# Routing inside the delta rule, fixed areas for the experts' tokens, and an expert pipeline over tiles

## What is computed

```python
# 1. delta rule, per batch and head, over 768 positions
k_n = k / (norm(k) + 1e-6)
y[t] = q[t] @ state
state += beta[t] * outer(k_n[t], v[t] - k_n[t] @ state)
# x = y as 3072 tokens x 384
# 2. mixture of experts, 8 experts, one for each token
logits = x @ w_gate;  e = argmax(logits)
out = softmax(logits)[e] * sigmoid(x @ w_output_gate)[e] * (relu(x @ w1[e]) @ w2[e])
# 3. last layer
h = max(out @ m1, out @ m2, out @ m3);  result = h @ w_out
```

## Time and profile before

| | us |
|---|---|
| median of 3 runs (lowest, highest) | 1198.79 (1197.86, 1202.87) |
| the profiled execution | 1203.62 |
| its span, first to last instruction | 1201.9 |
| TensorE busy, VectorE busy in the span | 1030.9, 480.0 |
| delta rule, to the last router product | 0 to 501 |
| routing, scatter and the first tile's load | 501 to 560.5 |
| experts | 560.5 to 873 |
| last layer | 873 to 1202 |

### The profile page before, as it was taken

The page is one execution under the profiler, slowest core; times in us unless marked ns, Lnnn a source line. Parts: engine busy times, 40 slices in busy tenths (PEclk is TensorE's granted clock), DMA queues, the critical chain, the costliest instruction groups (busy, mean ns, idle before and its releaser), DMA issues. The chain is left out here.

```text
span 1201.9 us, 31001 instructions
## 1 busy us (share of the span) xinstructions
PE 1030.9 (86%) x13236; PEld 895.3 (74%) x13237; DVE 480.0 (40%) x922; ACT 365.8 (30%) x732; POOL 327.6 (27%) x226
## 2 busy tenths in 40 slices
PE   1699999999999999603988998899959999999999
PEld 1588788888887787502877887788848887888888
DVE  3355555555555554332234323433334233242322
ACT  0245445555545455200212212212222122121211
POOL 2222333232333220084255045531630001000000
PEclk9979999999999999755999999999979999999999
DMA  8712122122111110043333244412320101100000
GB/s 267 270 29 60 29 56 55 43 60 60 29 56 38 40 34 3 1 156 127 138 116 113 85 144 137 144 42 103 111 66 20 45 28 33 33 20 27 7 20 27
DMA packets 59389, 86.29 MB, mean 72 GB/s; under 512 B 29200, under 2 KB 54288, under 8 KB 56720
## 3 DMA queue, kind: packets, MB, share of 16 engines
q1 hardware_dynamic: 53616, 48.46, 12.7%
q0 software_dynamic: 5664, 36.18, 8.9%
HBM read 61.82 MB, written 22.81 MB: 70 GB/s over the span
## 5 line engine op out<-in xcount | busy, mean ns | idle before, releaser
L1009 PE MATMUL hb<-early,last_h 128*128 128x512 f32 x648 | 203.8, 396 | 4.7 <-ACT o_sb L1123 3.6
L1009 PEld LDWEIGHTS hb<-early,last_h 128*128 128x128 f32 x648 | 120.5, 189 | 30.8 <-ACT o_sb L1123 2.7
L1009 PE MATMUL hb<-early,last_l 128*128 128x512 f32 x324 | 126.9, 392 | 0.0
L480 DVE TENSOR_TENSOR p<-bank,cf 128x512 f16<-128x512 f32 x96 | 66.0, 688 | 46.3 <-PE bank L283 46.0
L283 PEld LDWEIGHTS bank<-t,n_hi 64*64 64x64 f16 x2688 | 66.7, 111 | 22.8 <-issue 7.4
L931 POOL TENSOR_TENSOR late<-w_raw,late 128x3072 fp32r<-128x3072 f32 x8 | 59.7, 7459 | 73.6 <-DVE late L918 73.6
L1147 DVE TENSOR_TENSOR m<-hb,m 128x512 f32<-128x512 f32 x36 | 24.9, 692 | 131.4 <-PE hb L1009 131.4
L283 PE MATMUL bank<-t,n_hi 64*64 64x64 f16 x2688 | 72.0, 195 | 5.1 <-issue 4.3
L1009 PE MATMUL ob<-wo_h,early 128*128 128x384 f32 x288 | 74.2, 335 | 0.0
L881 ACT ACTIVATE h_sb<-h_bank 128x512 f32<-128x512 f32 x28 | 16.8, 598 | 186.5 <-PE h_bank L792 186.5
L792 PE MATMUL y_acc<-early,ht_h 128*128 128x384 f32 x240 | 63.4, 345 | 11.3 <-DVE ht_l L903 11.3
(11 more groups left out here) (157 smaller groups left out, 2258.8 us busy)
## 6 DMA issues: line engine op xcount, KB each, us to landing
w_raw<-w POOLq DMA_DIRECT2D x14, 1536.0 KB, 6.9
kq_t<-qh SPq DMA_DIRECT2D x24, 256.0 KB, 3.3
x_sorted<-zeros SPq DMA_DIRECT2D x32, 192.0 KB, 1.9
x_in<-x_sorted SPq DMA_DIRECT2D x29, 192.0 KB, 2.3
y_sorted<-y_sb SPq DMA_DIRECT2D x28, 192.0 KB, 1.9
k_raw<-kt_in SPq DMA_DIRECT2D x24, 192.0 KB, 3.3
k_own<-kh SPq DMA_DIRECT2D x24, 192.0 KB, 3.3
v_in<-vh SPq DMA_DIRECT2D x24, 192.0 KB, 3.5
```

The costliest lines, as they stand in the source:

```text
L480: dve.tensor_tensor(p16[st][:], pb, mask_of(lv), ALU.mult).then_inc(prod_out[st], 1)
L1009: ins = pe.matmul(out, a[x], b[y], start=first and i == 0, stop=last and i == 2, skip_group_check=True)
```

## The change

- **Routing per tile.** Behind `lg` the chain gets three positions: 15 `rank`, 16 `slot`, 17 `send`. VectorE finds the chosen expert of the tile right behind `lg`; TensorE ranks the tokens with two small f16 products (against a triangle, and against ones with the counts so far); VectorE takes the row number and adds to the counts; POOL scatters the tile from `y_tile`, which has two buffers now. `x_all` and its copies are gone, as is `route_and_sort`.
- **Fixed areas.** Expert `e` owns 24 blocks of rows of `x_sorted`, wherever the others end, so that a row is known before all tokens are counted. All 192 blocks are zeroed, in 24 DMAs of 8 blocks (1.57 MB) by SyncE, two of them ahead of the first weights and two after each step's loads, each waiting for the one before. The table is made at the end of the delta rule from one product with the counts.
- **Router products** have 16 columns: `wr` is not padded.
- **The first weight split** is cut in 6 pieces for each part and stands in `NORM` (10, 11, 12) of steps 2 to 7; the loads of the second expert's weights are at `NORM` 13 of step 10.
- **Within a slot** the chain goes through the oldest step first.
- **Experts.** The output product of tile `g - 1` is done in two halves around the transposes of hidden tile `g`. y tiles leave three blocks later (`LEAD`). VectorE makes one high part ahead of the first tile and one behind. The gates are computed at the start of this stage. The loop over experts is written out.

```diff
-    CHAIN = {..., 12: ("yt", 0), 14: ("lg", 0)}
-    NORM = {1: [0], 2: [1], 3: [2], 5: [3], 6: [4], 7: [5], 8: [6], 9: [7, 8], 10: [9]}
+    CHAIN = {..., 12: ("yt", 0), 14: ("lg", 0),
+             15: ("rank", 0), 16: ("slot", 0), 17: ("send", 0)}
+    NORM = {1: [0], 2: [1], 3: [2], 4: [10], 5: [3], 6: [4], 7: [5], 8: [6], 9: [7, 8], 10: [9], 12: [11], 13: [13], 14: [12]}
 # walk
-                for of, off in ((a, 0), (c, SLOTS), (b, 2 * SLOTS)):
+                for of, off in ((b, 2 * SLOTS), (c, SLOTS), (a, 0)):
 # SyncE, in the loop over steps, behind load_qv(k)
+            zero_area(2 * k - 2)
+            zero_area(2 * k - 1)
 # TensorE
                 elif k >= 1:
-                    pe.wait_ge(logit_out[st], k)
+                    pe.wait_ge(routed[st], 5 * k - 1)      # ks of the next step
-                    ins = pe.matmul(out[:, X:X + P], y_t[st][:, c, :], wr[:, c, :], ...)
+                    ins = pe.matmul(out[:, X:X + 2 * E], y_t[st][:, c, :], wr[:, c, :], ...)
+            elif what == "rank":
+                pe.wait_ge(chosen_ready[st], k + 1)
+                if 2 * k + st >= 1:
+                    pe.wait_ge(counted_ready, 2 * k + st)
+                pe.matmul(out[:, X + P - E:X + P], tri16, chosen[:, 2 * k + st, :], start=True, stop=False, ...)
+                pe.matmul(out[:, X + P - E:X + P], ones16, counted[:], start=False, stop=True, ...).then_inc(rank_done[st], 1)
 # VectorE, behind the copy of the logits: reduce max, compare, reduce max, compare -> chosen; then
+            elif what == "slot":
+                dve.wait_ge(rank_done[st], k + 1)
+                dve.tensor_tensor(place[st][:], yb[st][:, X + P - E:X + P], chosen[:, to, :], ALU.mult).then_inc(routed[st], 1)
+                dve.tensor_reduce(slot_f[:, to:to + 1], place[st][:], AX.X, ALU.add).then_inc(routed[st], 1)
+                dve.tensor_copy(rows_at[:, to:to + 1], slot_f[:, to:to + 1]).then_inc(slot_ready[st], 1)
+                dve.tensor_tensor(counted[:], counted[:], chosen[:, to, :], ALU.add).then_inc(counted_ready, 1)
 # POOL
-            if what == "yt":
-                pool.tensor_copy(x_all[:, 2 * k + st, :], y_tile[st][:]).then_inc(x_out[st], 1)
+            if what == "send":
+                pool.wait_ge(slot_ready[st], k + 1)
+                pool.wait_ge(area_zeroed, 16 * (to + 1))
+                if k >= 1:
+                    pool.wait_ge(rows_sent[st], 16 * k)
+                pool.indirect_dma_start(xs, bass.IndirectOffsetOnAxis(ap=rows_at[:, to:to + 1], axis=0),
+                                        y_tile[par][st][:], None).then_inc(rows_sent[st], 16)
 # experts, TensorE
+        def tile(e, par, g, first):
+            if first:
+                pe.wait_ge(weights.lo_ready[0], e + 1)
+            hidden(par, g)
+            transpose_x(g + 1)
+            ...
+            of = 1 - par if first else par
+            pe.wait_ge(ht_lo[1], g)
+            output(of, 0)
+            transpose_h(g)
+            output(of, 1).then_inc(y_done, 1)
 # experts, VectorE
+            if first:
+                high_part(e, par, 0)
             ... rectify, split_x(g + 1), split_h(g, 0), output(g), split_h(g, 1) ...
+            if first:
+                high_part(e, par, 1)
```

More of the change, by code:

```diff
@@ L132, in attention_and_router @@
     z = single("z", [P, NP, 2, D], F32)
-    y_tile = single("y_tile", [P, X], F32)
+    y_tile = double("y_tile", [P, X], F32)
     y_t = single("y_t", [P, KX, P], F32)
     zeros = sb("zeros", [P, X], F32)
+    best = sb("best", [P, 2], F32)
+    score = single("score", [P, E], F32)
+    top = sb("top", [P, 2], F32)
+    place = single("place", [P, E], F32)
+    rows_at = sb("rows_at", [P, TILES], U32)
+    counted = sb("counted", [P, E], F16)
+    more = sb("more", [P, E, TILES], F32)
+    blocks = sb("blocks", [P, E], F32)
+    sums = sb("sums", [P, E, E], F32)
+    ends = sb("ends", [P, E], F32)
+    begins = sb("begins", [P, E], F32)
+    logits, chosen, slot_f, shift, table = routing
     bank = [[ctx.enter_context(nc.psum_tensor(f"bank{st}{i}", [P, 512], F32)) for i in range(3)] for st in range(2)]
@@ L593, in norm @@
                 pool.tensor_tensor(ksq[:], keys, keys, ALU.mult).then_inc(squares, 1)
+            elif part == 13 and k == STEPS - 2:
+                for i, w in enumerate((w1, w2)):
+                    pool.wait_ge(weights.lo_ready[i], 1)
+                    pool.dma_start(weights.raw[i][:], w[1]).then_inc(weights.raw_again[i], 16)
         pool.wait_ge(const_in, 64)
@@ L746, in experts @@
-def experts(nc, ctx, sems, cf, table, xs, ys, weights, w1, w2, w_in, w_out):
+        for st in range(2):
+            pool.wait_ge(rows_sent[st], 16 * STEPS)
+def experts(nc, ctx, sems, cf, routing, gate, slots, xs, ys, weights, w1, w2, w_in, w_out):
     def sem(name):
@@ L768, in experts @@
     y_sb = sb("y_sb", [P, X])
+    logits, chosen, slot_f, shift, table = routing
+    lg, og = logits[:, :, 0:E], logits[:, :, E:2 * E]
+    best_of = sb("best_of", [P, TILES])
+    spread = sb("spread", [P, TILES, E])
+    exps = sb("exps", [P, TILES, E])
+    picked = sb("picked", [P, TILES, E])
+    denom = sb("denom", [P, TILES])
+    z_gate = sb("z_gate", [P, TILES])
+    exp_gate = sb("exp_gate", [P, TILES])
+    product = sb("product", [P, TILES])
+    moved = sb("moved", [P, E])
     h_bank = [ctx.enter_context(nc.psum_tensor(f"h_bank{i}", [P, 512], F32)) for i in range(2)]
@@ L785, in experts @@
     y_sent = sem("y_sent")
+    gate_step = sem("gate_step")
+    exps_ready = sem("exps_ready")
     ident = cf[:, CF_ID:CF_ID + P]
@@ L793, in three, with of_experts @@
         return ins
[L795 to L813 removed]
+    def of_experts(eng, tile):
+        begin = 0
+        for e in range(E):
+            end = eng.value_load(table[0:1, 1, e:e + 1], min_val=1, max_val=MAXB)
+            tile(e, e % 2, begin, True)
+            with eng.Fori(begin + 1, end) as g:
+                tile(e, e % 2, g, False)
+            begin = end
+        return end
+    passed_pool, passed_sp = sem("passed_pool_x"), sem("passed_sp_x")
     block = ctx.enter_context(nc.Block())
@@ L909, in before @@
-        def before(e, par):
-            if isinstance(e, int) and e == E - 1:
-                for i in range(2):
-                    dve.wait_ge(weights.raw_again[i], 16 * E)
-                    dve.tensor_copy(weights.last[i][0], weights.flat_raw(i)[:, 0:KX * F2]).then_inc(weights.last_hi[i], 1)
-            else:
-                for i in range(2):
-                    dve.wait_ge(weights.raw_again[i], 16 * e + 16)
-                    dve.tensor_copy(splits[1 - par][i][0], weights.flat_raw(i)).then_inc(weights.hi_ready[i], 1)
@@ L920, in _, with over_e, gates_first @@
-        dve.memset(y_sb[:, 0:1], 0.0).then_inc(y_sent, 1)
+            split_h(g, 0)
+            if not (first and e == 0):
+                output(g)
+            split_h(g, 1)
+            if first:
+                high_part(e, par, 1)
+        def over_e(x):
+            return x.unsqueeze(2).broadcast_to((P, TILES, E))
+        def gates_first():
+            dve.tensor_reduce(best_of[:], lg, AX.X, ALU.max).then_inc(gate_step, 1)
+            dve.tensor_tensor(picked[:], chosen[:], og, ALU.mult).then_inc(gate_step, 1)
+            dve.wait_ge(gate_step, 1)
+            dve.tensor_tensor(spread[:], lg, over_e(best_of[:]), ALU.subtract).then_inc(gate_step, 1)
+            dve.wait_ge(gate_step, 2)
+            dve.tensor_reduce(z_gate[:], picked[:], AX.X, ALU.add).then_inc(gate_step, 1)
@@ L921, in _ @@
+        dve.memset(y_sb[:], 0.0).then_inc(y_out, LEAD)
+        dve.memset(best_of[:, 0:1], 0.0).then_inc(xt_done, 1)
+        dve.wait_ge(xt_done, 1)
+        gates_first()
         split_x(0)
-        of_experts(dve, body, before)
+        gates_last()
+        total = of_experts(dve, tile)
+        output(total)
     @block.gpsimd
```

409 lines of the change are left out of this document (199 added, 210 removed).

## The result

The changed kernel takes 1250.12 us (median of 4 runs, 1243.99 to 1254.38) against 1200.83 for the kernel before on the same chip: ratio 1.0408, 95% interval 1.0356 to 1.0461, **slower by 4.1%**. Forecast were 1191 us and a range of 1140 to 1235. The profiled execution took 1254.38, its span is 1252.7 us.

What follows compares the result with a forecast made beforehand. TensorE was taken to set the pace. Span 1201.9 - 46 - 38 - 2 + 6 - 6 + 61 - 2 + 19 = 1193.9, with the median 3.1 below the span giving 1191 us; range 1140 to 1235.

Steps and rivals of the forecast that it cites:

- The gap: Between delta rule and experts: only the last tile's routing is left before the first expert product; about 46 us saved.
- The expert pipeline: Experts: splitting the previous output product around the transposes covers TensorE's waits for the hidden tile; about 38 us saved.
- POOL's new wait: Delta rule, steps 2 to 10: `send` ahead of `kb` delays q and v, nine gram stalls of 6.6 to 6.8; 61 us added.
- Rival 1: Delta rule: the gram stalls don't come, POOL reaching `kb` in time or q and v already landed; 1113 us, chance 0.13.
- The clock behind each stall: Delta rule: about 4.6 us at half clock after each of nine stalls loses 2.1 each; 19 us added.
- Rival 2: First half of windows 2 to 10: clock stays down long behind each stall, 6.5 us instead of 2.1; 1231 us, chance 0.18.
- the forecast's own sign of being wrong: Gram product waits for nothing, stalls under 5 or over 8 us, or clock low for more than 6 us behind one.
- The start: Start of kernel: two large zero writes replace 40 small DMAs, first weights come sooner, hole and half clock go; 6 us saved.
- The zero areas: Delta rule: 24 writes of 1.57 MB, 5.8 us each on the DMA engines, called free because next loads had over 15.
- Rival 3: Zero writes starve the engines: a quarter of 24 bring a 2.59 us hole and 2 us of clock; 1218 us, chance 0.09.
- VectorE, router products: Delta rule: more small VectorE operations and split pieces add 6 us; router products of 16 columns save 2.
- The last layer: After the experts: not touched by the change, so its time stays; 0 us.

Runs made afterwards that it cites:

- e4: Changed kernel with 24 pairs of unread products on TensorE ahead of the first stream's wait for q and v in steps 2 to 10; 1233.79 us.
- e2: Changed kernel with only one block instead of eight zeroed per write after the first five tile indices; 1210.55 us, ratio 1.0086.
- e3: Changed kernel with both edits, `send` one slot later and few zeros as in e2; 1141.08 us, ratio 0.9504.
- e1: Changed kernel with `send` one slot later (18 instead of 17), so POOL makes `kb` of the other stream first; 1185.30 us, ratio 0.9842.
- e5: Kernel before plus only 20 zero writes of 1.57 MB, two a step in steps 2 to 11, into memory nothing reads; 1246.98 us, ratio 1.0376.
- e9: e8 with seven of eight tail writes moved behind POOL's start in the experts, no pad, routing tiles at the other end of on-chip memory; 1128.60 us.
- e8: e1 without area zeroing: areas of 25 blocks, eight indirect writes of 128 zero rows behind the last tokens, and a 64-byte pad tile; 1149.26 us.
- e10: Kernel before plus only 20 zero writes of 0.79 MB, four blocks instead of eight each; 1211.01 us, ratio 1.0089.

## Why the prediction was wrong, point by point

- **The gap** (-46): -45.0. Right; the wait for x_in is 9.5 us where "about 10" was forecast.
- **The expert pipeline** (-38): -39.9. Right; a tile lasts 9.69 us (653.09 to 662.78 for its hidden product and the next) against 9.6.
- **POOL's new wait** (+61, nine times 6.6 to 6.8): the mechanism, its place and its count are right, and the size was 52.8 us (5.9 each). Rival 1 fell.
- **The clock behind each stall** (+19): 16 to 25 by e4 and the trace. Rival 2 fell by its price. But the forecast's own sign of being wrong, a clock low for more than 6 us behind a stall, came in four of nine (6.2 to 6.8 us): 4.6 us was too short a stretch.
- **The start** (-6): the first router copy is at 92.4 instead of 97.4, 5 earlier. Right.
- **"The zero areas. ... Free, by that cover."** This is the step that failed. The cover that it named (the next loads have over 15 us) was real but answers another question: whether the loads come late. The zero writes hold up TensorE itself, and it depends on none of their data: its blocks of instructions come late (below). Measured: -40 by e2 against the changed kernel, -44 by e3 against e1, +46 by e5 on the kernel before. All the area zeros together cost 55 us of the delta rule (47 and 8, below), most of the 59 us between forecast and result. Rival 3 had the mechanism, from the one hole of 2.59 us, but at 27 us and a chance of 0.09. It took a quarter of the writes to bring a hole; in fact nearly every pair brings one or two. Its evidence against, 267 and 270 GB/s in the first 60 us, was a mean over 30 us slices. It hid a stretch of 405 GB/s from 52 to 56 us, right ahead of the hole, and earlier than that few products run.
- **VectorE, router products** (+6 and -2): too small. In e9, where neither stalls nor area zeros are left, the delta rule from the first router copy to the last lasts 421.6 us against 404.0, +17.6 where +4 was forecast. TensorE waits 4.6 us for `chosen` in front of the rank products; the rest is spread over hand-overs that I have not taken apart.
- **The last layer** ("not touched, and its time stays"): +5.8 us, from where its operands lie in the on-chip memory (e9). An allocation is part of a change even where its code is not.

The terms for the delta rule, as the experiments give them: 64 for the order and its clock (last router copy 631.3 against 567.2 in e1), 47 for the zero writes of tile index 5 and up (e1 to e3), 8 for the rest of the zeros (e3 to e8), 11 for the new VectorE and TensorE work less the better start; in all 130, as measured. Against the forecast the order and its clock came 14 cheaper (78), the zeros 55 dearer, VectorE, the router products and the start 13 dearer (-2).

**What TensorE lacks in the holes** is in the traces: its instructions. They come over the same DMA engines, in blocks of 16,384 bytes on a queue of their own. First that queue over the whole span of the changed kernel (packets, MB, share of the engines), then all DMA queues from 220 to 225 us and from 225 to 226, around the start of the hole at 224.88 to 227.93:

```profile
q8 instruction: 98, 1.61, 0.5%
...
q1 hardware_dynamic: 1495, 1.69, 100.4%
...
q1 hardware_dynamic: 141, 0.19, 51.8%
q8 instruction: 1, 0.02, 5.5%
```

While the zero write fills the engines no block moves. One moves at 225.56 to 226.44, as the write ends, and TensorE goes on 1.49 us after it has landed. The other holes are like it. From 92 to 631 us 72 blocks come for some 18,600 of TensorE's instructions, about one for every 256. All 17 holes over 0.9 us there, beside the nine gram stalls and two waits at the end of the delta rule, begin at the same place of such a block, a multiple of 256 instructions apart (within one), and end 1.3 to 1.6 us after a block has landed; the nine gram stalls stand at nine different places of a block. In e5 it is 15 of 16, 35.8 us in all, in e10 10 of 11, 12.8 us. The hole of 2.59 us in the kernel before is one of them. In e5 the blocks behind the holes start 3.4 to 6.7 us after TensorE has entered the block before; in the kernel before the median is 1.8 us. So that TensorE waits for a late block of instructions is shown; that the block waits behind the packets of the write is read from the order in time, since no record tells when it was asked for.

In the experts, where loads of the same 1.57 MB run, TensorE has no such hole. There it needs few instructions, and six blocks are enough from 650 to 900 us:

```profile
700.00:750.00 50.00, 50.00 (x277) 45.39 (x276) 20.07 (x30) 11.87 (x21) 18.22 (x6) 1.00 0.40 138
```

277 products in 50 us against 1187 in the earlier trace rows.

**Still open.** What about the place of the operands makes the products 7 ns slower is not shown; 64 bytes are not it, and the addresses of the kernel before are not needed.

## What to carry to other kernels

Ask of a bulk transfer not only whether the next load is covered, but what it does to an engine that runs a thousand small instructions in 50 us: here writes of 1.57 MB at 400 GB/s cost 2.3 us each with no data dependence at all, because the instructions come over the same engines, and writing only the rows that are read cost nearly nothing. When an instruction with a late operand goes into an in-order queue, look at what stands directly behind it and follow that to the bottleneck; one slot was worth 65 us. And read "issue" as "not seen": it hid a late load at one line and a late block of instructions at the other, and only the DMA queues by the microsecond, or an experiment, tell them apart.

## What the runs showed of the hardware that was not expected

- A pair of 1.57 MB DRAM writes at about 400 GB/s leaves TensorE idle once or twice, for 1 to 3.4 us in the changed kernel and up to 4.6 in e5, in either order of the program; pairs of 0.79 MB do so less (+11 us for 20 writes against +46).
- TensorE's instructions came in blocks of 16,384 bytes, about one for every 256 instructions, over the same DMA engines; it stood still from the end of one block until 1.3 to 1.6 us after a late next one had landed.
- Half clock stood behind the hole of 3.05 us (0.50 in 230 to 232) and for 3.9 to 6.8 us behind stalls of some 6 us, where it cost 1.8 to 2.8 us each.
- Float32r products of 128x512 took 402 instead of 395 ns when their operands lay elsewhere in the on-chip memory, which made the last layer 5.8 us longer.
